# Logits by a different operand order: transposed attention rows as the stationary operand, and no folding product

## The chip, the cores and the metric

The kernel runs on one core of a Trainium2 chip. The time is the device time of the whole program in microseconds (us). In the profile the engines are PE (TensorE matmuls), PEld (TensorE weight loads), DVE (VectorE), ACT (ScalarE), POOL (GpSimd) and SP (which issues most of the DMAs).

## What is computed

Three stages follow each other. Attention with keys and values averaged over groups of 8 positions gives x (4608 tokens x 512); a soft mixture of 8 experts with 4 slots each routes tokens by `logits = x @ phi` (512 x 32); a dense layer with a softmax, a norm and an output product ends it.

```python
k_p = k.reshape(B, H, Sp, pool, D).mean(axis=3)      # B=8, H=8, S=576, D=64, Sp=72
v_p = v.reshape(B, H, Sp, pool, D).mean(axis=3)
scores = scale * np.matmul(q, k_p.transpose(0, 1, 3, 2))
attn = exp(scores - max); attn = attn / (sum + 1e-09)
x = np.matmul(attn, v_p)                             # then heads side by side: N x 512
...
logits = x @ phi                                     # N x 32
d = exp(logits - logits.max(0)); d /= d.sum(0)       # over the tokens
slot_input = d.T @ x
h = np.maximum(slot_input[e] @ w1[e], 0.0); slot_out[e] = h @ w2[e]
c = softmax(logits, over the slots); y = c @ slot_out
h = y @ w_in ... out = ln @ w_out
```

## The kernel before

x is never built. For each batch the kernel forms vphi, the product of the pooled values with phi, and takes the logits of a token as its attention row times vphi. An attention row of a token holds, for four pairs of heads, `PAIR` = 147 columns (a one, and for each head 72 probabilities and a tiny constant), 588 in all, cut into `NB` = 5 blocks of 128 (the last has 76).

A batch has 576 tokens: four tiles of 128 and one (t = 4) in which the 64 left over stand twice, half of the heads each. Tiles are numbered on through the batches. `steps` runs one step for each tile: the first batch written out, six batches in a hardware loop (two per turn), one last step, and then a tail written by hand. In the step of tile t, TensorE does, in program order, the scores of tile t + 2 (`scores`), pieces of the routing statistics of the batch before (`lmax_t`, `mb_t`, `dat_t`, `datT_t`, `slot_t`), the logits of tile t - 1 and the transposes of the attention rows of tile t (`aT_t`). Engines work in the order in which the code is written, and wait for each other by semaphores.

The part around the change, before:

- `wphi_t`: once a batch, four products phi_pair (stationary, 32 columns) by vpad (moving, 147 columns), each in its own quarter of the array's columns; ScalarE copies the four results into the wide matrix wphi (`wphi_evac`). `vphi_t` then transposes wphi in five pieces, and VectorE copies and sums them into vphi (`vphi_evac`, three instructions).
- `lt_t`: for each tile, five products with vphi (stationary, 32 columns) and the transposed attention rows aT (moving, 128 columns), spread over the four column quarters of the array, so the logits come out transposed and in four partial sums. ScalarE copies them (`lt_evac`).
- `l_t`: one product of that copy (stationary, 128 columns) with `fold4` (moving, 32 columns), which transposes back and adds the four parts. VectorE copies the result into c_all (`logit_evac`).

ScalarE's order in a step is: other copies, `lt_evac` of tile t - 1, the exponentials `exps` of tile t + 2 (they need VectorE's subtraction of the maximum, `sub_max`), and the two copies `aT_evac` of tile t. The logits of a tile need `aT_evac` of it.

Of the kernel before, what the change touches and what calls it, by code (L numbers as in the profile page):

```python
# [31 lines left out]
ALU = mybir.AluOpType  # L32
# [29 lines left out]
NB = len(BLOCKS)  # L62

# [15 lines left out]
def build(nc, q, k, v, phi, w1, w2, w_in, w_out, g_ln, out):  # L79
    with ExitStack() as ctx:  # L80
# [41 lines left out]
        wphi = bump("wphi", [P, PAIRS * PAIR])  # L122
        kblk = [bump("kblk0", [P, PAIRS, 2 * SP])]
        assert place[0] >= p1 + 2 * HALF
        lt = [bump(f"lt{i}", [P, P]) for i in range(2)]
        datT = bump("datT", [SP, 2, P])
        assert place[0] >= p1 + 2 * HALF
# [3 lines left out]
        vpad = bump("vpad", [P, PAIRS, PAIR])  # L131
# [7 lines left out]
        vphi = [bump(f"vphi{i}", [P, NB, SLOTS]) for i in range(2)]  # L139
# [12 lines left out]
        dlog = bump("dlog", [P, TILES, SLOTS])  # L152
        dexp = bump("dexp", [P, TILES + 1, SLOTS])
# [9 lines left out]
        assert (WO_EARLY - 1) * 4 * DM <= size([P, QCOLS]) and WO_EARLY == FC - 3  # L163
        for e, t in ((FC - 1, 1), (FC, 3)):
            assert wo0 + e * 4 * DM <= attn0 + 4 * (t + 1) * PAIRS * PAIR
# [5 lines left out]
        assert wo0 + size([P, FC, DM]) + HALF // 4 <= attn0 + (attn_end - attn0) // 2  # L171
        for e, t in ((4, 1), (7, 3)):
            assert wo0 + size([P, FC, DM]) + HALF * e // FC <= attn0 + (attn_end - attn0) // 2 + 4 * (t + 1) * PAIRS * PAIR
# [51 lines left out]
        b_v72, b_aT, b_lt, b_tail, b_head = ps[2], ps[3:5], ps[5], ps[6], ps[7]  # L225
# [24 lines left out]
        def weights(e, layer):  # L250

            n = 2 * e + layer
            return half(n % 10), sem(f"w_in{n % 10}"), {8: 16 * 2, 9: 16 * 4, 10: 16 * (1 + MC)}.get(n, 16 * (n // 10 + 1))
# [32 lines left out]
        def l_bank(tile):  # L286

            return ps[1] if isinstance(tile[0], int) and tile[0] == B - 1 and tile[2] == 4 else b_lt
# [42 lines left out]
        def vpad_half(hh):  # L331
            return vpad[hh * D:(hh + 1) * D, :, 1 + hh * HEAD:1 + hh * HEAD + SP]
# [51 lines left out]
        def _(sp):  # L384
# [64 lines left out]
            sp.wait_ge(sem("vphi_ps"), B)  # L449
            load_w(3, 0)  # L450
            sp.wait_ge(sem("s_ps"), B * TILES - 1)
            load_out(0, WO_EARLY - 1, 0)
            sp.wait_ge(sem("s_ps"), B * TILES)
            sp.wait_ge(sem("wphi_ps"), B)
            load_out(WO_EARLY - 1, WO_EARLY, 0)
# [3 lines left out]
            load_out(WO_EARLY, FC - 1, 1)  # L459
            sp.wait_ge(sem("dat_ps"), dat_count(B - 2, 3))  # L460
            load_out(FC - 1, FC, 1)
            sp.wait_ge(sem("dat_ps"), dat_count(B - 2, TILES - 1))
            load_part(9, 0, 2)
            sp.wait_ge(sem("lt_ps"), B * TILES)
            load_part(8, 1, 4)
            for t, a, e in ((1, 2, 4), (3, 4, 7), (4, 7, 8)):
                sp.wait_ge(sem("dat_ps"), dat_count(B - 1, t))
                load_part(9, a, e)
# [42 lines left out]
        def _(pool):  # L511
# [4 lines left out]
            pool.memset(vpad[:, :, :], 0.0).then_inc(sem("zeros"), 1)  # L516
            pool.memset(wphi[:, :], 0.0).then_inc(sem("zeros"), 1)
            pool.memset(kblk[1][:, :, :], 0.0).then_inc(sem("pool_set"), 1)
            pool.wait_ge(sem("pool_set"), 2)
            pool.wait_ge(sem("zeros"), 2)  # L520
# [118 lines left out]
        def _(act):  # L639
# [14 lines left out]
            def wphi_evac(b):  # L654

                act.wait_ge(sem("wphi_ps"), b + 1)
                for j in range(PAIRS):
                    g = 32 * GROUP[j]
                    last = copy(wphi[g:g + 32, PAIR * j:PAIR * (j + 1)], b_head[g:g + 32, 0:PAIR])
                last.then_inc(sem("wphi_sb"), 1)  # L660

# [5 lines left out]
            def lt_evac(tile):  # L667
                act.wait_ge(sem("lt_ps"), num(tile) + 1)
                o, i = lt[bit(tile)][:, :], l_bank(tile)[:, 0:P]
                if tile[2] == TILES - 1:  # L670
                    o, i = o.rearrange("p (a n) -> p a n", a=2), l_bank(tile)[:, 0:LEFT][:, None, :].to_broadcast([P, 2, LEFT])
                copy(o, i).then_inc(sem("lt_sb"), 1)
# [47 lines left out]
            act.wait_ge(sem("zeros"), 2)  # L720
# [3 lines left out]
            wphi_evac(0)  # L724
            exps((0, 0, 2))

            def step(b, par, t, first, last):
# [3 lines left out]
                if t == 5:  # L731
                    wphi_evac(b + 1)
# [12 lines left out]
                if first:  # L745
                    if t != 1:
                        lt_evac(ahead(b, par, t - 1))
# [4 lines left out]
                    if t == 1:  # L752
                        lt_evac(ahead(b, par, t - 1))
                    exps(ahead(b, par, t + 2))
                    return
                lt_evac(ahead(b, par, t - 1))
# [10 lines left out]
            lt_evac(last_tile(1))  # L767
# [3 lines left out]
            lt_evac(last_tile(2))  # L771
# [6 lines left out]
            lt_evac(last_tile(3))  # L778
            lt_evac(last_tile(4))
# [139 lines left out]
        def _(dve):  # L919
# [63 lines left out]
            def logit_evac(tile):  # L983
                dve.wait_ge(sem("l_ps"), num(tile) + 1)
                dve.tensor_copy(batch_logits(tile[0])[:, tile[2], :], l_bank(tile)[:, P:P + SLOTS]).then_inc(sem("l_sb"), 1)
# [791 lines left out]
```

## Time and profile before

| | |
|---|---|
| median of 3 runs | 441.24 us (440.08 to 441.43) |
| the profiled execution | 440.7 us, span of its instructions 438.9 us |
| busy share of the span | PE 94%, PEld 73%, DVE 70%, ACT 54%, POOL 56% |
| granted TensorE clock, mean | 0.996 of full speed |
| DMA | 91.68 MB, mean 209 GB/s |

A busy share is the union of the instructions' durations on an engine. TensorE's products overlap each other (one lasts about 0.3 us and the next starts about 0.1 us after it), so for TensorE the time from one start to the next is what an instruction takes of the engine. The span has three parts: attention and routing up to about 160 us, the experts up to about 200, and the last layer.

### The profile page before, as it was taken

What the parts mean: (1) busy time and instruction counts of PE and PEld (TensorE: products, weight loads), DVE (VectorE), ACT (ScalarE), POOL (GpSimd) and SP (SyncE); (2) the same over time, 40 slices, a digit from 0 to 9 for tenths busy, and PEclk for the clock granted to TensorE, in tenths of its full rate; (3) what the DMA queues carried; (4) which work ended last, traced back from release to release, by engine and by line L of the source; (5) the groups of instructions that cost most, each with busy time, mean ns of one, the idle gap of its engine ahead of it and who ended that gap; (6) DMA issues with size and microseconds to landing.
All of it is one profiled execution on the core that took longest, in us unless ns stands there. A gap on an engine that the chain in (4) does not pass through costs nothing.

```text
span 438.9 us, 9468 instructions
## 1 busy us (share of the span) xinstructions
PE 413.2 (94%) x3303; PEld 319.1 (73%) x3303; DVE 307.3 (70%) x543; ACT 238.8 (54%) x497; POOL 243.8 (56%) x346
## 2 busy tenths in 40 slices
PE   6788989899899889999899999999999999999997
PEld 6666777677777664455687887888888888888886
DVE  4878788787887747355889976777777777777211
ACT  1457775667756542153777655656555656555310
POOL 2579988888883311020143375757677666676540
PEclk8999999999999999999999999999999999999999
DMA  8847789769695699996001676677666666766732
GB/s 322 331 126 307 309 326 390 288 246 419 247 433 191 231 397 346 431 424 284 1 7 43 131 143 117 130 141 139 134 133 114 135 132 134 143 135 115 157 73 48
DMA packets 79212, 91.68 MB, mean 209 GB/s; under 512 B 67024, under 2 KB 67408, under 8 KB 74448
## 3 DMA queue, kind: packets, MB, share of 16 engines
q1 hardware_dynamic: 74016, 82.07, 60.9%
q10 hardware_dynamic: 5168, 9.24, 6.3%
q8 instruction: 16, 0.26, 0.2%
q14 instruction: 12, 0.10, 0.1%
HBM read 66.13 MB, written 9.44 MB: 172 GB/s over the span
## 4 chain that ended last, share of the span: by engine, by line
PE 75%; DVE 12%; ACT 5%; issue 4%; POOL 3%; DMA 1%; ACTq 0%; DVEq 0%
PE banks L1697 14%; PE banks L1698 14%; PE banks L1699 14%; PE banks L1313 5%; PE banks L1560 3%; PE banks L1669 3%; PE banks L1582 3%; PE banks L1356 2%; PE banks L1416 2%; DVE smax L960 2%; DVE attn L966 2%; DVE ssum L973 2%; PE banks L1387 2%; PE banks L1380 2%; ACT aT L641 1%
## 5 line engine op out<-in xcount | busy, mean ns | idle before, releaser
L1697 PE MATMUL banks<-wo_hi,uh 128*128 128x512 f32 x280 | 110.5, 395 | 0.1
L1698 PE MATMUL banks<-wo_lo,uh 128*128 128x512 f32 x280 | 110.0, 393 | 0.0
L1699 PE MATMUL banks<-wo_hi,ul 128*128 128x512 f32 x280 | 109.1, 390 | 0.0
L609 POOL TENSOR_TENSOR ul<-u_col,uh 128x1024 fp32r<-128x1024 f32 x30 | 71.9, 2397 | 18.6 <-ACT uh L641 18.2
L876 ACT ACTIVATE sq<-u,st 128x1024 f32<-128x1024 f32 x36 | 41.5, 1152 | 39.9 <-DVE u L1198 39.9
L533 POOL TENSOR_TENSOR attn<-attn,srec 128x576 f32<-128x576 f32 (+1 forms) x40 | 43.1, 1078 | 35.5 <-DVE srec L978 35.5
L1697 PEld LDWEIGHTS banks<-wo_hi,uh 128*128 128x128 f32 x280 | 52.6, 188 | 12.7 <-DVE ul L1215 0.5
L1699 PEld LDWEIGHTS banks<-wo_hi,ul 128*128 128x128 f32 x280 | 52.5, 188 | 12.1
L1698 PEld LDWEIGHTS banks<-wo_lo,uh 128*128 128x128 f32 x280 | 52.6, 188 | 11.3
L1198 DVE SCALAR_TENSOR_TENSOR u<-banks,ex 128x1024 f32<-128x1024 f32 x35 | 42.7, 1223 | 24.5 <-ACT ex L867 24.4
L1188 DVE TENSOR_REDUCE st<-banks 128x1 f32<-128x1024 f32 x35 | 42.6, 1216 | 18.3 <-PE banks L1669 18.3
L867 ACT ACTIVATE ex<-banks,st 128x1024 f32<-128x1024 f32 x35 | 39.0, 1115 | 18.4 <-DVE st L1188 17.7
L641 ACT ACTIVATE uh<-u_col 128x1024 fp32r<-128x1024 f32 x30 | 31.7, 1058 | 30.2 <-DMA u_col<-u_blk 16.3
L1313 PE MATMUL banks<-kblk,qb 128*128 128x144 f32 x256 | 40.6, 303 | 5.3 <-DVE attn L966 2.4
L1313 PEld LDWEIGHTS banks<-kblk,qb 128*128 128x128 f32 x256 | 34.0, 194 | 10.1 <-DVE attn L966 4.7
L1229 DVE TENSOR_SCALAR osb<-banks,rs 128x512 f32<-128x512 f32 x35 | 25.9, 741 | 19.5 <-PE banks L1699 19.5
L665 ACT ACTIVATE attn<-attn 128x576 f32<-128x576 f32 (+1 forms) x40 | 25.4, 636 | 25.5 <-DVE attn L966 25.1
L1208 DVE STREAM_TRANSPOSE u_blk<-u 128x1024 f32<-128x1024 f32 x30 | 37.4, 1246 | 1.9
L595 POOL TENSOR_SCALAR st<-st 128x1 f32<-128x1 f32 x36 | 6.9, 191 | 52.5 <-ACT sq L876 52.2
L374 POOL TENSOR_TENSOR vraw<-vraw 128x1152 f32<-128x1152 f32 (+1 forms) x14 | 29.5, 2108 | 7.4 <-DMA vraw<-in_v 7.4
L960 DVE TENSOR_REDUCE smax<-banks 128x8 f32<-128x576 f32 (+1 forms) x40 | 27.2, 680 | 8.4 <-PE banks L1313 8.4
L973 DVE TENSOR_REDUCE ssum<-attn 128x8 f32<-128x584 f32 (+1 forms) x40 | 27.8, 694 | 6.7 <-ACT attn L665 6.4
(179 smaller groups left out, 692.0 us busy)
## 6 DMA issues: line engine op xcount, KB each, us to landing
wslot<-in_moe_w SPq DMA_DIRECT2D x13, 2048.0 KB, 13.2
u_col<-u_blk SPq DMA_DIRECT2D x240, 64.0 KB, 2.2
vraw<-in_v SPq DMA_DIRECT2D x8, 1152.0 KB, 5.1
out<-osb ACTq DMA_DIRECT2D x32, 256.0 KB, 2.8
kraw<-in_k SPq DMA_DIRECT2D x7, 1152.0 KB, 7.2
qb<-in_q SPq DMA_DIRECT2D x7, 1152.0 KB, 7.6
wslot<-in_moe_w SPq DMA_DIRECT2D x4, 512.0 KB, 7.2
win<-in_moe_w_in SPq DMA_DIRECT2D x4, 512.0 KB, 22.1
```

Of the source, the lines that this page charges most:

```text
L533: pool.tensor_tensor(a, a, per_head(srec[bit(tile)], t)[:, :, :, None].to_broadcast([P, tile_pairs(t), 2, SP]), ALU.mult) \
L609: pool.tensor_tensor(ul[par][:, :, :].rearrange("p c (q t) -> p (c q) t", q=4), v, uh[par][:, :, :].bitcast(F32).rearrange("p c (q t) -> p ...
L867: act.activation(ex[par][:, :, :], h_banks(par), ACT.Exp, bias=st[k % STATS]["nmax"][:, :], accum_out=st[k % STATS]["den"][:, :]).then_inc ...
L876: act.activation(sq[par][:, :], u[k % URING][:, :], ACT.Square, scale=-float(FF), bias=st[k % STATS]["usum"][:, :], accum_out=st[k % STATS ...
L973: dve.tensor_reduce(per_head(ssum[par], t), head_sums(tile[1], t), AX.X, ALU.add).then_inc(sem("ssum"), 1)
L1188: dve.tensor_reduce(st[k % STATS]["nmax"][:, :], h_banks(k % 2), AX.XY, ALU.max, negate=True).then_inc(sem("nmax"), 1)
L1198: dve.scalar_tensor_tensor(u[k % URING][:, :].rearrange("p (a n) -> p a n", a=2), h_banks(par), 1.0, ex[par][:, :, :], ALU.mult, ALU.mult, ...
L1208: dve.transpose(u_blk[slot][:, :, :, k % 2, :].rearrange("p c q t -> p (c q) t"), u[k % URING][:, :].rearrange("p (b f) -> p b f", f=BLK)) \
L1313: last = pe.matmul(s_view[:, j, 0:2 * SP], q_cols(par, t, j), kblk[par][:, j, :], start=True, stop=True)
L1697: pe.matmul(ps[4 + par], uh[par][:, c, :], wo_hi[:, c, :], start=(c == 0), stop=False)
L1698: pe.matmul(ps[4 + par], uh[par][:, c, :], wo_lo[:, c, :], start=False, stop=False)
L1699: last = pe.matmul(ps[4 + par], ul[par][:, c, :], wo_hi[:, c, :], start=False, stop=(c == FC - 1))
```

## The change

The two operands of both products change places, and what was only there to bring the result back falls away.

- `vphi_t` takes a block of 128 columns of vpad as the stationary operand and phi_pair (32 columns) as the moving one, so vphi comes out as it is needed. For that vpad is stored with room between the pairs (`VPAD` = 147 + 128 columns a pair) so that a block of 128 can be cut at any of the five block positions; a block over two pairs takes two products that accumulate: eight in all. `wphi_t`, `wphi_evac` and the transposes are gone, and `vphi_evac` is one copy.
- The new `l_t` takes aT (128 columns) as the stationary operand and vphi (32 columns) as the moving one: five products that accumulate in one place, in the full array. For t = 4, where a tile is 64 tokens, there are twelve products in two halves of the array's columns; both halves compute the same logits, since the copies of the 64 tokens are wanted twice. The folding product, `lt_evac` and VectorE's `logit_evac` are gone; ScalarE copies the logits straight into c_all (`l_evac`).
- Some tiles move in SBUF, and a few loads of weights at the end of attention are cut in other pieces and wait for other semaphores.

```diff
-            def wphi_t(b):
+            def vphi_t(b):
                 pe.wait_ge(sem("vT_sb"), b + 1)
                 if not (isinstance(b, int) and b == 0):
                     pe.wait_ge(sem("vphi_sb"), b)
-                for j in range(PAIRS):
-                    g = 32 * GROUP[j]
-                    last = pe.matmul(b_head[g:g + 32, 0:PAIR], phi_pair[:, j, :], vpad[:, j, :], start=True, stop=True, tile_position=(0, g))
-                last.then_inc(sem("wphi_ps"), 1)
-
-            def vphi_t(b):
-
-                pe.wait_ge(sem("wphi_sb"), b + 1)
-                for n in range(1, 4):
-                    pe.transpose(b_head[:, 32 + P * (n - 1):32 + P * n], wphi[:, P * n:P * (n + 1)], ident[:, :])
...
+                for k in range(NB):
+                    pairs = [j for j in (k - 1, k) if 0 <= j < PAIRS]
+                    for j in pairs:
+                        last = pe.matmul(b_head[:, SLOTS * k:SLOTS * (k + 1)], vpad_block(j, k), phi_pair[:, j, :], start=(j == pairs[0]), stop=(j == pairs[-1]))
+                last.then_inc(sem("vphi_ps"), 1)
...
-                if t == 4:
-                    for n in range(2 * LNB):
-                        k, hh, g = n // 2, n % 2, n % 4
...
+                if t == TILES - 1:
+                    parts = [(k, hh) for hh in range(2) for k in range(LNB)]
+                    for i, (k, hh) in enumerate(parts):
                         m = BLOCKS[NB - 1] if k == LNB - 1 else P
...
+                        for c in (0, LEFT):
+                            last = pe.matmul(l_bank()[c:c + LEFT, :], aT[bit(tile)][0:m, k, LEFT * hh:LEFT * (hh + 1)], vphi[par][0:m, k + LSKIP * hh, :],
+                                             start=(i == 0), stop=(i == len(parts) - 1), tile_position=(0, c))
                 else:
                     for k, m in enumerate(BLOCKS):
-                        g = k % 4
-                        last = pe.matmul(b_lt[32 * g:32 * (g + 1), 0:P], vphi[par][0:m, k, :], aT[bit(tile)][0:m, k, :],
-                                         start=(k < 4), stop=(k + 4 >= NB), tile_position=(0, 32 * g))
-                last.then_inc(sem("lt_ps"), 1)
-
-            def l_t(tile):
-
-                pe.wait_ge(sem("lt_sb"), num(tile) + 1)
-                pe.matmul(l_bank(tile)[:, P:P + SLOTS], lt[bit(tile)][:, :], fold4[:, :], start=True, stop=True).then_inc(sem("l_ps"), 1)
+                        last = pe.matmul(l_bank(), aT[bit(tile)][0:m, k, :], vphi[par][0:m, k, :], start=(k == 0), stop=(k == NB - 1))
+                last.then_inc(sem("l_ps"), 1)
...
-            def lt_evac(tile):
-                act.wait_ge(sem("lt_ps"), num(tile) + 1)
...
+            def l_evac(tile):
+                act.wait_ge(sem("l_ps"), num(tile) + 1)
+                copy(c_all[:, bass.ds(tile[0], 1), tile[2], :].rearrange("p o s -> p (o s)"), l_bank()).then_inc(sem("l_sb"), 1)
...
             def vphi_evac(b, par):
                 dve.wait_ge(sem("vphi_ps"), b + 1)
-                dve.tensor_copy(vphi[par][:, 0, :], b_head[:, 0:32])
-                dve.tensor_reduce(vphi[par][:, 1:4, :], b_head[:, 32:32 + 3 * P].rearrange("p (k g s) -> p k s g", k=3, g=PAIRS), AX.X, ALU.add)
-                dve.tensor_copy(vphi[par][0:BLOCKS[4], 4, :], b_head[0:BLOCKS[4], 64 + 3 * P:96 + 3 * P]).then_inc(sem("vphi_sb"), 1)
+                dve.tensor_copy(vphi[par][:, :, :], b_head[:, 0:NB * SLOTS].rearrange("p (k s) -> p k s", k=NB)).then_inc(sem("vphi_sb"), 1)
```

TensorE's program in the loop, from the transposes of tile t = 4 to those at the end of a batch. Names are outputs and inputs, the numbers behind them are buffers, and the shape is that of the output. Before:

```order
L1352 MATMUL banks<-ident,attn 128x64 x6
L1387 MATMUL banks<-fold_50,lt_69 128x32
L1425 MATMUL banks<-ident,dat 72x128 x2
L1323 MATMUL banks<-vpad,phi_pair 32x147 x4
L1297 REGISTER_ALU
L1313 MATMUL banks<-kblk_75,qb_72 128x144 x4
L1434 MATMUL banks<-v_1_83,datT 32x64 x8
L1364 ISA
L1375 MATMUL banks<-aT_78,vphi_80 32x64 x6
L1356 MATMUL banks<-ident,attn 128x128 x4
```

The kernel before goes on from there, to the end of the batch:

```order
L1356 MATMUL banks<-ident,attn 76x128
L1387 MATMUL banks<-fold_50,lt_68 128x32
L1340 MATMUL banks<-ident,vT_77 72x128 x4
L1330 MATMUL banks<-ident,wphi 128x128 x3
L1331 MATMUL banks<-ident,wphi 128x32
L1332 MATMUL banks<-ident,wphi 76x64
```

The same place of the changed program:

```order
L1386 MATMUL banks<-ident,dat 72x128 x2
L1274 REGISTER_ALU
L1290 MATMUL banks<-kblk_66,qb_62 128x144 x4
L1395 MATMUL banks<-v_0_81,datT 32x64 x8
L1333 ISA
L1343 MATMUL banks<-vphi_80,aT_79 64x32 x12
L1326 MATMUL banks<-ident,attn 128x128 x4
L1326 MATMUL banks<-ident,attn 76x128
L1310 MATMUL banks<-ident,vT_76 72x128 x4
L1301 MATMUL banks<-phi_pair,vpad 128x32 x8
```

The folding products (L1387), the four products of L1323 and the five transposes of wphi are gone; twelve products of 64 x 32 stand where six of 32 x 64 stood, and eight of 128 x 32 stand at the end of the batch.

ScalarE's program in the step of t = 5 of a batch (the first tile of the next one), from the copy datT to the copies of aT. Before:

```order
L641 ACTIVATE datT<-banks 72x256
L641 ACTIVATE wphi<-banks 32x147 x4
L641 ACTIVATE lt_69<-banks 128x128
L664 REGISTER_ALU
L665 ACTIVATE attn<-attn 128x4x2x72
L675 ISA
L641 ACTIVATE aT_78<-banks 128x512
L675 REGISTER_ALU
L641 ACTIVATE aT_78<-banks 76x128
```

The changed one:

```order
L643 ACTIVATE datT<-banks 72x256
L643 ISA
L643 ACTIVATE c_all<-banks 128x32
L658 REGISTER_ALU
L659 ACTIVATE attn<-attn 128x4x2x72
L666 ISA
L643 ACTIVATE aT_78<-banks 128x512
L666 REGISTER_ALU
L643 ACTIVATE aT_78<-banks 76x128
```

The wphi copies are gone, and the copy of the logits stands where the copy lt stood, ahead of the exponentials (`attn<-attn`).

## Rows read from the trace of the kernel before

**Rows 1.** Table by stretch, attention loop: window, its length, each engine's busy us, clock, DMA

```profile
38.00:145.50 107.50, 99.91 (x1280) 78.44 (x1280) 86.64 (x205) 72.76 (x210) 85.33 (x65) 1.00 0.76 303
```

**Rows 2.** Timeline of TensorE, first steps of a batch: start us, length us, what [idle before]

```profile
75.18 0.60 PE L1380 MATMUL banks<-aT,vphi 128*32 128x128 f32 x10
75.71 0.77 PE L1356 MATMUL banks<-ident,attn 128*128 128x128 f32 x5
76.31 0.31 PE L1387 MATMUL banks<-fold,lt 128*128 128x32 f32 x2
77.11 0.71 PE L1309 MATMUL banks<-kblk,qb 128*64 128x144 f32 x8 [0.49 <-DVE attn L966]
78.47 0.63 PE L1380 MATMUL banks<-aT,vphi 128*32 128x128 f32 x10 [0.65 <-ACT aT L641]
...
80.50 1.24 PE L1313 MATMUL banks<-kblk,qb 128*128 128x144 f32 x8 [0.22 <-issue]
```

**Rows 3.** Timeline of TensorE, the rest of the same batch

```profile
82.19 0.60 PE L1380 MATMUL banks<-aT,vphi 128*32 128x128 f32 x10
82.73 0.77 PE L1356 MATMUL banks<-ident,attn 128*128 128x128 f32 x5
...
83.78 0.96 PE L1416 MATMUL banks<-attn,dexp 128*32 128x147 f32 x24
84.67 1.25 PE L1313 MATMUL banks<-kblk,qb 128*128 128x144 f32 x8
85.85 0.63 PE L1380 MATMUL banks<-aT,vphi 128*32 128x128 f32 x10
86.41 0.41 PE L1352 MATMUL banks<-ident,attn 64*128 64x64 f32 x6
86.84 0.41 PE L1387 MATMUL banks<-fold,lt 128*128 128x32 f32 x2
87.09 0.39 PE L1425 MATMUL banks<-ident,dat 128*72 128x128 f32 x2
...
87.79 1.25 PE L1313 MATMUL banks<-kblk,qb 128*128 128x144 f32 x8
...
89.25 0.42 PE L1375 MATMUL banks<-aT,vphi 128*32 128x64 f32 x12
89.60 0.76 PE L1356 MATMUL banks<-ident,attn 128*128 128x128 f32 x5
...
90.57 0.61 PE L1340 MATMUL banks<-ident,vT 128*72 128x128 f32 x4
91.01 0.49 PE L1330 MATMUL banks<-ident,wphi 128*128 128x128 f32 x3
91.43 0.24 PE L1331 MATMUL banks<-ident,wphi 32*128 32x32 f32 x1
...
91.79 0.39 PE L1313 MATMUL banks<-kblk,qb 128*128 128x144 f32 x1
```

**Rows 4.** Timeline of TensorE, four products of the last stage's preparation

```profile
205.45 1.08 PE L1628 MATMUL banks<-fold,so 128*128 128x32 f32 x8 [0.20 <-DVE so L1172]
```

**Rows 5.** The same line by itself: duration ns min/median/max, first and last start

```profile
L1628 PE MATMUL banks<-fold,so x8: 276/276/297, 205.4 to 206.3; 128*128 128x32 f32 x8
```

**Rows 6.** Timeline of ScalarE, the exponentials of the batch's second step

```profile
75.82 0.28 ACT L641 ACTIVATE lt<-banks 128x128 f32<-128x128 f32 x1 [0.98 <-PE banks L1380]
77.09 0.68 ACT L665 ACTIVATE attn<-attn 128x576 f32<-128x576 f32 x1 [1.00 <-DVE attn L966]
```

**Rows 7.** Timeline of VectorE, the copies into vphi

```profile
73.86 0.19 DVE L989 COPY vphi<-banks 128x32 f32<-128x32 f32 x1 [0.29 <-PE banks L1332]
...
74.53 0.75 DVE L973 TENSOR_REDUCE ssum<-attn 128x8 f32<-128x584 f32 x1
```

**Rows 8.** Timeline of TensorE, end of the first batch and of the attention stage

```profile
36.34 0.73 PE L1356 MATMUL banks<-ident,attn 128*128 128x128 f32 x5 [0.55 <-POOL attn L533]
...
158.43 0.43 PE L1396 MATMUL banks<-ident,lmax 128*32 128x128 f32 x8 [0.40 <-DVE lmax L997]
```

More of the change, by code:

```diff
@@ L62 @@
 NB = len(BLOCKS)
+VPAD = PAIR + P
 LPAIRS = PAIRS // 2
@@ L121, in build @@
         kp = bump("kp", [P, PAIRS, SP])
-        wphi = bump("wphi", [P, PAIRS * PAIR])
         kblk = [bump("kblk0", [P, PAIRS, 2 * SP])]
-        assert place[0] >= p1 + 2 * HALF
-        lt = [bump(f"lt{i}", [P, P]) for i in range(2)]
+        vphi = [bump("vphi0", [P, NB, SLOTS])]
+        place[0] = p1 + 2 * HALF
         datT = bump("datT", [SP, 2, P])
+        dlog = bump("dlog", [P, TILES, SLOTS])
+        dexp = bump("dexp", [P, TILES + 1, SLOTS])
         assert place[0] >= p1 + 2 * HALF
@@ L138, in build @@
         aT = [bump(f"aT{i}", [P, NB, P]) for i in range(2)]
-        vphi = [bump(f"vphi{i}", [P, NB, SLOTS]) for i in range(2)]
+        vphi.append(bump("vphi1", [P, NB, SLOTS]))
         assert place[0] <= attn_end + HALF
@@ L162, in build @@
         WO_EARLY = (attn0 - wo0) // (4 * DM)
-        assert (WO_EARLY - 1) * 4 * DM <= size([P, QCOLS]) and WO_EARLY == FC - 3
-        for e, t in ((FC - 1, 1), (FC, 3)):
-            assert wo0 + e * 4 * DM <= attn0 + 4 * (t + 1) * PAIRS * PAIR
+        assert WO_EARLY == FC - 2 and wo0 + FC * 4 * DM <= attn0 + 4 * 2 * PAIRS * PAIR
         wten = bump("wten", [P, 4 * FF])
@@ L168, in build @@
         place[0] = attn_end
[L171 to L173 removed]
+        ten = attn0 + (attn_end - attn0) // 2 - (wo0 + size([P, FC, DM]))
+        assert 4 * 4 * DM <= ten
+        for e, t in ((6, 1), (8, 3)):
+            assert e * 4 * DM <= ten + 4 * (t + 1) * PAIRS * PAIR
         wnine = at("wnine", [P, 4 * FF], F32, attn_end)
@@ L284, in last_tile, with l_bank @@
             return B - 1, 1, t
-        def l_bank(tile):
-            return ps[1] if isinstance(tile[0], int) and tile[0] == B - 1 and tile[2] == 4 else b_lt
+        def l_bank():
+            return b_l[:, 0:SLOTS]
         def tile_pairs(t):
@@ L746, in step @@
                     if t != 1:
-                        lt_evac(ahead(b, par, t - 1))
+                        l_evac(ahead(b, par, t - 1))
                     if t == 4:
@@ L1060, in step @@
                         slot_acc(b - 1, 1 - par)
-                logit_evac(ahead(b, par, t - 1))
                 if t == 5:
@@ L1461, in step @@
                     dat_t(b - 1, 1 - par, (4,))
-                if t == 1 and first:
-                    wphi_t(b)
-                if t == 5 and first:
-                    wphi_t(b + 1)
                 if not (last and t + 2 >= TILES):
@@ L1476, in step @@
                     vphi_t(b)
+                    pe.wait_ge(sem("aT_sb"), 2)
                     aT_t(tile)
-                lt_t(before, first and t == 1)
+                l_t(before, first and t == 1)
                 if t == 2 and not first:
@@ L1486, in step @@
                     dat_t(b - 1, 1 - par, (0, 1))
-                l_t(before)
                 if t == 2 and first:
@@ L1494, in step @@
                         datT_t(b - 1)
-                if t == 4 and not last and not first:
-                    wphi_t(b + 1)
                 if t == 5:
```

98 lines of the change are left out of this document (32 added, 66 removed).

## The prediction

> **What bounds the kernel now.** I read the table by stretch first: in the attention loop TensorE is busy 99.9 of 107.5 us at full clock, VectorE 86.6, the others less [rows 1]. All that the change touches lies in this stage. Busy time of TensorE can hide waits, though, so I read its timeline next, from start to start. In the shown batch (one turn of the loop holds two) it waits visibly in three places only: 0.49 us for VectorE's subtraction, 0.65 for ScalarE's copy aT, 0.22 at the next scores [rows 2]. From 80.50 to 91.79 it goes from one piece of work to the next with no idle shown [rows 2, 3]. So what a change adds to TensorE's work there comes out in full, and what it takes from VectorE or ScalarE is worth only what it shortens of those waits.
>
> **The unit prices.** In the trace each product of the program (not a transpose) has two rows, so the five products of a tile are ten rows. The new product, 128 columns of f32 stationary and 32 moving, stands in the trace in just this form: four of them in a row last 1.08 us as eight rows, one row lasting 0.28 [rows 4, 5], so the rows follow each other every (1.08 - 0.28)/7 = 0.114 us. Five products take 1.14 us, the eight of vphi 16 x 0.114 = 1.82. The old group of five takes 0.54 from its start to the next work (82.19 to 82.73), since four column quarters work at once; at 85.85 it takes 0.56 [rows 3]. Both hold the step back from narrow columns to the full array. I price such a change of shape from two neighbours: four transposes take 90.57 to 91.01, 0.11 each; three more, followed by one of another row shape, take 0.42, so the change costs 0.42 - 0.33 = 0.09 [rows 3].
>
> The twelve products of t = 4 are not in the trace in their form. They are 24 rows in 12 pairs, the two column halves together. Upper bound for a pair: the scores in the same two halves, four pairs with 144 moving columns, 0.71 us with about 0.28 for the last, so (0.71 - 0.28)/3 = 0.14 a pair [rows 2]. Lower bound: half of the 0.114, if the time goes with the stationary columns, 64 instead of 128. With 32 moving columns the form is nearer to that one; I take 0.057, hence 0.68 for twelve.
>
> The Trainium skill ("TensorE: Matmul & The Clock Gate", Back-to-back issue gap) gives some 81 ns for a sustained stream of weight loads and 128-column products, where the row above has 114. By the page's figure the change would come out otherwise; I price that as a rival and keep the row for the sum.
>
> **The change step by step, for one batch of the loop.** I go through TensorE's places in order of time.
>
> 1. First two tiles, up to 80.50. The logits group at 75.18 follows narrow work: it costs the change of shape earlier, 0.09, and 1.14 instead of 75.18 to 75.71: +0.69. The folding product is gone: -0.25 (its place 86.84 to 87.09) [rows 2, 3]. That is +0.44, and the wait of 0.49 behind it takes it up if VectorE is earlier. It is: its three copies into vphi take 73.86 to 74.53, 0.67 [rows 7]; one copy costs at least the 0.19 of a fifth of its columns and at most those 0.67, so I take 0.25 and VectorE comes 0.4 sooner. The scores stay at about 77.1. The next group waits for ScalarE, where the exponentials (77.09, released by VectorE) stand ahead of the copy aT [rows 6]. There a new wait appears: the copy of the logits stands ahead of the exponentials, and the logits of this tile now end at 75.18 + 0.09 + 1.03 + 0.28 = 76.58; with a copy of 0.2 (bounds 0.19, the vphi copy of the same shape, and 0.28, the old one) the exponentials can start at 76.85, not 0.4 but 0.24 sooner. So the group at 78.47 starts at 78.23, takes 0.6 to 0.7 longer, and the 0.22 wait and one folding product (0.25) are given back: 80.4 to 80.5. No change; since the loop's other batch waits less there, I take +0.05.
> 2. Up to 84.67. The group at 82.19 follows narrow work: +0.69. From the transposes at 82.73 to 83.78 there are 1.05 us, for five transposes (0.60, as 75.71 to 76.31) and a change of shape (0.09) once the folding product and its wait for ScalarE's copy go [rows 2, 3]: -0.36. Sum +0.33.
> 3. Up to 87.79. The scores no longer end in a change of shape, -0.09. The group at 85.85 takes 1.14 for 0.56, and 0.09 to change to the half-row transposes: +0.67. Folding product -0.25. From datT (87.09) to the next scores 0.70 us go down to two transposes, 0.24, without the wphi products and their two changes of shape: -0.46 [rows 3]. Sum -0.13.
> 4. Up to 91.79. The t = 4 group, 0.35 from 89.25 to 89.60, becomes 0.68 + 0.18 for two changes of shape, +0.51. Transposes and folding product, 89.60 to 90.57, 0.97 to 0.60: -0.37. The transposes of wphi, 91.01 to 91.79, 0.78, against 1.82: +1.04 [rows 3]. Sum +1.18.
>
> The batch becomes 0.05 + 0.33 - 0.13 + 1.18 = 1.4 us longer. VectorE loses five small copies a batch and ScalarE four wphi copies; both are hidden behind TensorE already and bring nothing more.
>
> **Where it counts.** Six batches run in the loop: 8.5. In the first batch TensorE waits for POOL and VectorE in most steps, as at 36.34 (0.55 of idle) [rows 8], and that takes up the longer groups; behind that wait there are the vphi products, +1.04, less the place of one folding product, of which I take 0.14, a row or so, since nothing waits for it there: +0.9. In the tail after 145.5 four more groups follow. The first starts 0.24 sooner and is 0.7 longer, the next two add some 0.6 each and lose a folding product (0.25 each); the last (t = 4) adds 0.4 and must wait for ScalarE's copies of transposes that now come just before it. That is 0.5 + 0.3 + 0.3 + 0.4 plus about 0.6 of wait, against one wait that shrinks: before, 158.43 came after two folding products and two copies behind the last group [rows 8], and one product and one copy, 0.3 or so, go. I take +1.8. The expert stage and the last layer do the same work as before; the weight loads cut anew are tied to work that itself comes later, and attention gives them more time.
>
> Sum: 8.5 + 0.9 + 1.8 = 11.2 us on the profiled execution's own 440.7 (span 438.9), so 451.9. The median of the runs is 0.5 above that execution: **452.4 us**.
>
> **The rivals.**
>
> - *Forecast*: added TensorE time comes out as summed, 449.7 to 455. Chance 0.60.
> - *Waits give more back.* The 0.65 wait at 78.47 [rows 2] goes too, if the logits copy doesn't hold up the exponentials. For it: VectorE is 0.4 sooner. Against: the order on ScalarE. 7 x 0.65 = 4.6 less, about 447.8. With small errors of the unit price, 0.17.
> - *The half-column pairs go at 0.14*, not 0.057: 12 x 0.083 = 1.0 a batch, or ScalarE's late copies push out every step. Up to 8 us more, 455 to 460. Against: only 32 columns move. Chance 0.15.
> - *Faster than before*: weight loads of 128 columns run ahead under the work before, so the new rows follow more closely than 0.114. The trace has a hint: two rows of the folding product right behind transposes last 0.31 together, elsewhere 0.41 (76.31 and 86.84) [rows 2, 3], so the second came 0.10 earlier. It decides where 56 rows of this form a batch (four tiles of ten and sixteen for vphi) save the 1.4 us: at 1.4/56 = 0.025 less, 0.089 a row. At 0.08 a batch would be 0.034 x 56 - 1.4 = 0.5 shorter, some 3.5 us over seven batches with the tail even: 438. Against it: rows 4 and 5, a run of eight with every load free to run ahead, hold 0.114. Chance 0.05.
> - *No change*: all waits, 0.49 + 0.65 + 0.22 = 1.36 a batch, take up the 1.4. Steps 2 to 4 have no wait to do that. Chance 0.03.
>
> The page's 81 ns for such a stream would be the fourth of these, nearly at its 0.08. The same skill ("TensorEngine Tiling (Array Packing)", When to Use Tiling) advises what the kernel did before: with 32 moving columns, swap the operands and use four column tiles. By the rows that is right here, since five products take 0.54 so and 1.14 the other way.
>
> **How the numbers follow.** A range of 447.5 to 457 holds the forecast case, most of the second and the lower part of the third, a little over 8 in 10. What a measurement can tell from no change here is about 0.3%, 1.3 us. Faster 0.05, same 0.03, slower 0.92.
>
> **What would show it.** In the changed profile the logits rows (128 x 32) should start every 0.11, five products taking 1.1 us; the vphi products 1.8 us at the end of a batch; t = 4 about 0.7. A turn of the loop, two batches, should be 2.8 us longer. TensorE's wait for VectorE at the scores of t = 4 should be gone, the wait for ScalarE behind it should remain at about 0.6. Experts and last layer should keep their lengths. I am wrong if the rows of the new form come closer than 0.09, if the pairs take over 0.1, or if the steps from 80.50 on hold a wait that busy time hid from me.

## The result and the profile after

| | before | changed |
|---|---|---|
| median | 440.66 us (439.25 to 441.43, 4 runs) | 460.13 us (453.50 to 465.28, 4 runs) |
| ratio | | 1.0341, 95% interval 1.0248 to 1.0434 |
| profiled execution | 440.7 us, span 438.9 | 462.7 us, span 460.9 |
| mean granted clock of TensorE | 0.996 (profiled) | 0.966 (profiled); 0.989, 0.959, 0.978 in the others |

The ratio leaves out the two runs with the lowest clocks. The program is slower, as forecast. The two runs that the ratio keeps have a mean of 455.5 us, 3.1 above the forecast of 452.4 and inside the range; the median of all four lies 7.7 us above the forecast and above the top of the range, and the four times of one program lie 12 us apart. They are ordered by the clock: 453.50 us at 0.989, 457.55 at 0.978, 462.72 at 0.966, 465.28 at 0.959, some 3.9 us for each 0.01. So there are two things to read: what the change costs where the clock is full, and where the clock falls.

**Where the clock falls.** The row of the granted clock on the page of the changed kernel, over 40 slices of 11.5 us:

```profile
PEclk9985599999999998999999999999999999999999
```

and the same row of the kernel before:

```profile
PEclk8999999999999999999999999999999999999999
```

The table by stretch of the changed kernel (window, its length, busy us of PE, PEld, DVE, ACT, POOL, then the clock):

```profile
25.00:30.00 5.00, 3.65 (x30) 3.31 (x29) 3.57 (x6) 3.00 (x8) 2.52 (x2) 1.00 0.41 170
30.00:35.00 5.00, 5.00 (x29) 4.82 (x28) 2.84 (x6) 1.88 (x7) 4.38 (x4) 0.53 0.82 302
35.00:55.00 20.00, 20.00 (x115) 17.94 (x115) 8.49 (x19) 6.58 (x18) 11.23 (x10) 0.50 0.60 233
55.00:60.00 5.00, 5.00 (x60) 3.81 (x59) 1.78 (x3) 2.68 (x8) 2.30 (x1) 0.74 0.89 375
126.00:164.50 38.50, 37.38 (x439) 32.72 (x438) 26.88 (x54) 20.89 (x61) 22.39 (x19) 1.00 0.57 229
164.50:185.00 20.50, 18.00 (x229) 12.82 (x232) 8.69 (x21) 6.83 (x25) 3.61 (x6) 0.92 0.90 329
```

From about 30 to 57 us TensorE runs at the lower of its two levels, 1.2 instead of 2.4 GHz, and while it is there it is busy all the time: 5.00 of 5, 20.00 of 20. Reading busy shares alone one would see an engine at its limit; the counts give it away, 115 rows in 20 us against 439 in 38.5. TensorE's timeline there:

```profile
26.36 1.20 PE L1347 MATMUL banks<-vphi,aT 128*128 128x32 f32 x10
27.67 0.74 PE L1326 MATMUL banks<-ident,attn 128*128 128x128 f32 x5
29.65 1.71 PE L1290 MATMUL banks<-kblk,qb 128*128 128x144 f32 x8 [1.25 <-DVE attn L954]
31.16 2.18 PE L1347 MATMUL banks<-vphi,aT 128*128 128x32 f32 x10
33.27 0.59 PE L1322 MATMUL banks<-ident,attn 64*128 64x64 f32 x6
...
39.41 3.46 PE L1301 MATMUL banks<-phi_pair,vpad 128*128 128x32 f32 x16
42.68 2.27 PE L1290 MATMUL banks<-kblk,qb 128*128 128x144 f32 x8
```

What came before the fall: five logits products of the new form, five transposes, 1.25 us of waiting for VectorE's subtraction, and the first of eight rows of scores, which last 1.71 us together where the same eight take 1.25 at full clock. The next logits group takes 2.11 us to its successor (31.16 to 33.27), the vphi products 3.27.

**At full clock** the timeline of TensorE over a whole batch, the fifth of the loop's six:

```profile
126.00 1.23 PE L1290 MATMUL banks<-kblk,qb 128*128 128x144 f32 x8
127.16 0.42 PE L1357 MATMUL banks<-ident,lmax 128*32 128x128 f32 x8
127.51 1.30 PE L1347 MATMUL banks<-vphi,aT 128*128 128x32 f32 x10
128.65 0.74 PE L1326 MATMUL banks<-ident,attn 128*128 128x128 f32 x5
129.32 0.71 PE L1286 MATMUL banks<-kblk,qb 128*64 128x144 f32 x8
130.43 1.30 PE L1347 MATMUL banks<-vphi,aT 128*128 128x32 f32 x10 [0.39 <-ACT aT L643]
...
132.59 1.15 PE L1290 MATMUL banks<-kblk,qb 128*128 128x144 f32 x8
...
137.01 1.25 PE L1290 MATMUL banks<-kblk,qb 128*128 128x144 f32 x8
...
139.89 1.25 PE L1290 MATMUL banks<-kblk,qb 128*128 128x144 f32 x8
141.31 0.43 PE L1395 MATMUL banks<-v,datT 72*32 72x64 f32 x16 [0.17 <-ACT datT L643]
141.67 0.89 PE L1343 MATMUL banks<-vphi,aT 128*64 128x32 f32 x24
142.49 0.77 PE L1326 MATMUL banks<-ident,attn 128*128 128x128 f32 x5
...
143.53 1.87 PE L1301 MATMUL banks<-phi_pair,vpad 128*128 128x32 f32 x16
145.24 0.37 PE L1290 MATMUL banks<-kblk,qb 128*128 128x144 f32 x1
...
164.47 1.23 PE L1290 MATMUL banks<-kblk,qb 128*128 128x144 f32 x8
```

Starts are read here, and not lengths: a logits group goes from 127.51 to 128.65, 1.14 us; at t = 4 the group takes 0.82 (141.67 to 142.49); vphi takes 1.71 (143.53 to 145.24). The wait for VectorE at the scores of t = 4 [rows 2] is gone (129.32 has none), the one for ScalarE is 0.39, and there is a small new one, 0.17, for ScalarE's copy datT. In the kernel before, the batch of [rows 2] and [rows 3], also the first of its turn, began 1.42 us ahead of the first row of [rows 2], at 73.76:

```profile
73.76 1.25 PE L1313 MATMUL banks<-kblk,qb 128*128 128x144 f32 x8
```

It ended at 91.79 [rows 3]. So this batch takes 19.24 us for 18.03. The two batches of a turn take 38.47 (126.00 to 164.47) for 35.87 (73.76 to 109.63): +2.60 a turn, +1.3 a batch.

### The profile page after: what moved, and what is told of

The parts are those of the page before. It is cut to its first block, busy times and chain, and to the rows that moved or that the text cites. A ratio compares the mean times of both kernels' runs of the same rounds, so it can differ in the third digit from the quotient of the medians.

```text
span 460.9 us, 9460 instructions
## 1 busy us (share of the span) xinstructions
PE 442.5 (96%) x3343; PEld 355.8 (77%) x3343; DVE 299.4 (65%) x487; ACT 226.9 (49%) x465; POOL 243.9 (53%) x345
## 4 chain that ended last, share of the span: by engine, by line
PE 81%; DVE 8%; ACT 5%; issue 3%; POOL 2%; DMA 1%; ACTq 0%; DVEq 0%
PE banks L1648 13%; PE banks L1647 13%; PE banks L1649 13%; PE banks L1347 7%; PE banks L1290 6%; PE banks L1326 3%; PE banks L1510 3%; PE banks L1301 3%; PE banks L1619 3%; PE banks L1532 3%; PE banks L1377 3%; ACT aT L643 2%; DVE attn L954 2%; DVE smax L948 2%; PE banks L1343 2%
## 5 line engine op out<-in xcount | busy, mean ns | idle before, releaser
L1347 PEld LDWEIGHTS banks<-vphi,aT 128*128 128x128 f32 (+1 forms) x320 | 41.5, 205 | 8.8 <-ACT aT L643 6.0
L1290 PE MATMUL banks<-kblk,qb 128*128 128x144 f32 x256 | 42.6, 313 | 4.9 <-DVE attn L954 3.4
L1347 PE MATMUL banks<-vphi,aT 128*128 128x32 f32 (+1 forms) x320 | 44.0, 287 | 3.0 <-ACT aT L643 3.0
L1290 PEld LDWEIGHTS banks<-kblk,qb 128*128 128x128 f32 x256 | 36.2, 205 | 8.8 <-DVE attn L954 5.5
L643 ACT ACTIVATE c_all<-banks 128x32 f32 (+1 forms) x40 | 7.9, 197 | 68.4 <-PE banks L1347 56.8
```

What stands on the lines that cost most here:

```text
L643: return act.activation(o, i, ACT.Copy, scale=scale)
L1290: last = pe.matmul(s_view[:, j, 0:2 * SP], q_cols(par, t, j), kblk[par][:, j, :], start=True, stop=True)
L1347: last = pe.matmul(l_bank(), aT[bit(tile)][0:m, k, :], vphi[par][0:m, k, :], start=(k == 0), stop=(k == NB - 1))
```

## Experiments

Both theories below take it that the rows of the new form cost the summed 10 or 11 us and that the rest is the clock. **A**: the clock falls because TensorE sits idle at its waits. **B**: it falls because products that move only 32 columns for each load of 128 leave the array nearly empty, however busy the engine looks. Ratios are to the kernel before on the same chip, which had medians of 441.4, 441.8 and 440.2 us.

### Work in the gaps at the start

The kernel has a helper for such gaps, `keep_clock(bank, n)`, n transposes of the identity whose result nobody reads. Ten instead of three stand at t = 1 of the first batch, and twelve are new at t = 4.

```diff
                 if t == 1 and first:
-                    keep_clock(b_tail, 3)
+                    keep_clock(b_tail, 10)
+                if t == 4 and first:
+                    keep_clock(b_tail, 12)
```

> The changed kernel with 19 more transposes of the identity in the first batch, at two places where TensorE waits (about 1.0 us before the scores of tile 3 and 1.25 us before those of tile 6). Theory A (the clock falls after the first batch because TensorE sits idle there): no stretch at half clock behind 25 us, every run at 450 to 452.5, runs within 1 us of each other. Theory B (it falls because the new products keep the array nearly empty while its weight loads run): the fall comes later or in some runs only, times still scatter from 452 to 463. If the clock has nothing to do with the 8 us above the forecast, the time stays near 460.

Measured: 453.45 us (451.03 to 457.41), ratio 1.028 (1.020 to 1.0359). The clock is full from 25 to 60 us (33.54 busy of 35). Two runs at 0.996 take 451.11 and 451.03, two at 0.985 and 0.978 take 455.78 and 457.41. In the profiled one the clock now falls behind the loop. The row of its page, and below it TensorE's timeline there:

```profile
PEclk9999999999999966999999999999999999999999
```

```profile
158.31 1.30 PE L1347 MATMUL banks<-vphi,aT 128*128 128x32 f32 x10 [0.28 <-ACT aT L643]
...
161.38 2.34 PE L1347 MATMUL banks<-vphi,aT 128*128 128x32 f32 x10 [0.74 <-ACT aT L643]
163.53 1.31 PE L1326 MATMUL banks<-ident,attn 128*128 128x128 f32 x5
```

So there is a second weak place, the tail, where the same groups stand between waits. That work in the gap at the start helps is likely and not shown: two of four runs have a mean clock of 0.996, which none of the eight runs of the unedited changed kernel reaches, but the repeat below keeps its clock at the start without it. "Every run at 450 to 452.5", A's outcome, did not come true; the fall that comes later, or in some runs only, is B's. A repeat of the unedited changed kernel:

> The changed kernel once more, for the scatter. Both theories: runs between 450.5 and 466, and the later ones are those with the lower mean clock: about 4.3 us more for each 0.01 of clock lost.

Measured: 460.0 us (456.32 at clock 0.981 to 468.33 at 0.949), ratio 1.0422 (1.0344 to 1.0499). That is 3.8 us for each 0.01 of clock and not 4.3, and one run lies above the 466 expected. In this profile the clock stays up at the start and is 0.50 from 170 to 175 us, in the tail. Which weak place gives way changes from one execution to the next.

### The same products, moving four times the columns

The logits product of a full tile moves vphi four times over, 128 columns, into 128 columns of the same bank; nothing reads the last 96. Loads, waits and order stay.

```diff
-                        last = pe.matmul(l_bank(), aT[bit(tile)][0:m, k, :], vphi[par][0:m, k, :], start=(k == 0), stop=(k == NB - 1))
+                        last = pe.matmul(b_l[:, 0:4 * SLOTS].rearrange("p (r s) -> p r s", r=4), aT[bit(tile)][0:m, k, :],
+                                         vphi[par][0:m, k, :][:, None, :].to_broadcast([m, 4, SLOTS]), start=(k == 0), stop=(k == NB - 1))
```

> The changed kernel, in which the logits products of the four full tiles move vphi four times over (128 columns instead of 32) into spare columns of the bank; the output is the same. Rows of the form stay bound by their weight load, so 0.11 us each and 0 us on a batch at full clock. Theory B (a nearly empty array lets the clock fall): the clock stays up, 450 to 452.5 in every run. Theory A (idle time does it): nothing changes, half clock from about 30 to 57 us in some form, 453 to 465.

Measured: 453.53 us (452.71 to 454.10), ratio 1.0289 (1.0256 to 1.0322), clocks 0.992 to 0.996. More work, and the clock is at 0.992 or more in all four runs, where the changed kernel has 0.949 to 0.989 in eight. The median is 6.6 us below the changed kernel's; beside the two runs that the changed kernel's ratio keeps (455.5) it is 2.0 below. The rest is the runs at low clock, which the wide form does not have. TensorE's timeline at the place where the changed kernel's clock fell:

```profile
26.59 1.28 PE L1347 MATMUL banks<-vphi,aT 128*128 128x128 f32 x10
27.83 0.74 PE L1326 MATMUL banks<-ident,attn 128*128 128x128 f32 x5
29.82 1.25 PE L1290 MATMUL banks<-kblk,qb 128*128 128x144 f32 x8 [1.25 <-DVE attn L954]
30.90 1.28 PE L1347 MATMUL banks<-vphi,aT 128*128 128x128 f32 x10
```

The wait is the same 1.25 us, and the clock holds: 1.00 from 0 to 60 us. Waiting alone is not what lets it fall. The median is above the expected 450 to 452.5, since a wide group takes a little longer than a narrow one (a turn of the loop 38.9 us for 38.5) and a short dip in the tail stays, 0.67 from 170 to 175 us.

### Each half alone

Only `vphi_t` in its new form (eight products with vpad stationary, one copy), the logits, folding product and `lt_evac` as before:

> Only the vphi half of the change; the logits by four column quarters, copy and folding product as before. By the places of the forecast a batch of the loop takes +0.46 to +0.58 us against the kernel before (1.7 to 1.8 of products for 0.78 of transposes and 0.46 of wphi): 3.5 us over the whole, 444 to 445.5. A rival who holds that VectorE's shorter copy is what counts expects 439 to 440.

Measured: 444.61 us (443.26 to 446.26), ratio 1.0098 (1.0059 to 1.0137), clocks 0.988 to 0.999; a turn of the loop takes 36.62 us, +0.4 a batch. The expected 444 to 445.5 holds, and the rival's 439 to 440 does not.

Only the logits in their new form, wphi, its copies and its transposes as before:

> Only the logits half of the change; vphi by wphi and transposes as before. A batch of the loop takes +0.85 us: about 7 us with the tail, 447 to 449 at full clock; more, and scattered, if the clock falls at the start as in the full change. If the two halves add up, e3 and e4 together give the full change at full clock, +10 to +11.

Measured: 455.44 us (449.32 at 0.992 to 462.71 at 0.959); no ratio, since its runs lie too far apart. A turn takes 37.40, +0.77 a batch. The halves add up to 1.14 of the full change's 1.3, and the scatter comes with the logits half. In its profiled execution the clock dips to 0.70 from 45 to 50 us, and again in the tail. So the loop's first batch is a third weak place.

### The cost at full clock

The fills at the start, 13 more transposes at three places of the tail, and the wide form in the first batch and the tail only; the loop is that of the changed kernel.

```diff
             aT_t(last_tile(2))
+            pe.wait_ge(sem("v72_sb"), B)
+            keep_clock(ps[2], 5)
             l_t(last_tile(2))
...
+            keep_clock(ps[2], 3)
             l_t(last_tile(4))
+            keep_clock(ps[2], 5)
             datT_t(B - 2, ps[0])
```

> The changed kernel with fillers at the waits of the first batch (19 transposes of the identity) and of the tail (13), and with the logits products of the first and the last batch moving 128 columns (32 of them wanted); the loop is the changed kernel's own. Theory B (emptiness of the array together with waits lets the clock fall at both ends of the attention stage): all runs within 1.5 us at 450.5 to 452, clock 0.99 or more. If the fall could come in the loop as well, a run in four or so lies above 453.

Measured: 450.36 us (449.98 to 450.77), ratio 1.0207 (1.0178 to 1.0235), clocks 0.996 to 1.000. The scatter is gone, and this is about what the change costs when the clock does not fall; the fillers and the wide groups, which stand in its time too, cannot add much, since the two runs of the first experiment at 0.996 take 451.03 and 451.11. The table by stretch over the tail, filler included:

```profile
160.00:185.00 25.00, 24.16 (x347) 14.99 (x349) 12.37 (x29) 8.69 (x27) 2.69 (x6) 1.00 0.96 353
```

### The copy of the logits behind the exponentials

The rival "waits give more back" says that the copy into c_all holds the exponentials up. Here ScalarE takes them first, in the kernel of the last section.

```diff
-                l_evac(ahead(b, par, t - 1))
                 if not (last and t + 2 >= TILES):
                     exps(ahead(b, par, t + 2))
+                l_evac(ahead(b, par, t - 1))
```

> e6 with the exponentials ahead of the logits copy on ScalarE. The rival of the forecast (the wait for ScalarE at the second group goes if the copy doesn't stand in front): 4 us less than e6. My reading of the changed profile, where the exponentials start 0.08 us after VectorE is done: 0 to 0.5 us less.

Measured: 451.54 us (450.30 to 452.05), ratio 1.0221 (1.0189 to 1.0253), 1.2 above the unswapped one, for an expected 0 to 0.5 below. Most of the 1.2 is the clock. In the profiled execution, 452.05 us at 0.996, it falls for a short while in the loop's first batch, in spite of the fillers at both ends:

```profile
42.55 1.30 PE L1348 MATMUL banks<-vphi,aT 128*128 128x32 f32 x10 [0.45 <-ACT aT L643]
...
44.83 2.12 PE L1290 MATMUL banks<-kblk,qb 128*128 128x144 f32 x8
```

The eight rows of scores last 2.12 for 1.25. The swapped run at 0.999 takes 450.30, between the unswapped ones at 0.999, 450.17 and 450.56. So the swap gains nothing, and the loop of narrow products is not quite safe either.

TensorE's wait for ScalarE at the second group, in a batch that begins at 116.94, is 0.43 in place of 0.39. Why is seen on ScalarE's timeline there:

```profile
119.94 0.69 ACT L659 ACTIVATE attn<-attn 128x576 f32<-128x576 f32 x1 [3.04 <-DVE attn L954]
```

The row shows that even first in line the exponentials start 3.00 us into the batch; in the changed kernel it is 3.05, so the copy ahead of them costs 0.05. VectorE's subtraction sets the time, as its own timeline in the changed kernel says (batch from 126.00):

```profile
126.20 0.32 DVE L973 COPY vphi<-banks 128x160 f32<-128x160 f32 x1 [1.80 <-PE banks L1301]
126.44 0.75 DVE L961 TENSOR_REDUCE ssum<-attn 128x8 f32<-128x584 f32 x1
...
128.21 0.76 DVE L954 TENSOR_TENSOR attn<-banks,smax 128x576 f32<-128x576 f32 x1
```

The subtraction ends at 128.97, and ScalarE's copy and exponentials go at once:

```profile
128.95 0.20 ACT L643 ACTIVATE c_all<-banks 128x32 f32 x1 [2.98 <-PE banks L1347]
129.05 0.68 ACT L659 ACTIVATE attn<-attn 128x576 f32<-128x576 f32 x1
```

### Twice the logits products, narrow and wide

A stronger test of B in the loop, where TensorE waits little. In the kernel with the clock held up the loop moves 32 columns a product, and its clock stays up:

```profile
100.00:150.00 50.00, 48.66 (x574) 42.52 (x575) 34.52 (x71) 28.07 (x83) 33.27 (x27) 1.00 0.72 286
```

Now each full tile makes its five products twice, once into another part of the bank.

```diff
+                    for k, m in enumerate(BLOCKS):
+                        pe.matmul(b_l[:, 256:256 + SLOTS], aT[bit(tile)][0:m, k, :], vphi[par][0:m, k, :], start=(k == 0), stop=(k == NB - 1))
```

> e6 with the five logits products of each full tile made twice, the first time into unused columns of the bank (32 tiles, 320 more rows of 128 x 32). At 0.114 us a row, with about 2 to 4 us taken up by waits in the first batch and at the second tile of each batch: +32 to +35 us on e6. If weight loads could run ahead and a row took 0.08: +22 to +25.

Measured: 497.43 us (484.00 at clock 0.995 to 506.12 at 0.949). The run at 0.995 is 33.6 above the kernel without the second set, close to the sum at 0.114 a row. Then the same, with both sets moving 128 columns everywhere:

> e8 with both sets of logits products of the full tiles moving 128 columns instead of 32. A row then takes 0.123 us instead of 0.114, so the time at full clock is some 5 us above e8's fastest run, 487 to 490. Theory B (the emptiness of the array lets the clock fall): the clock stays at 0.99 or more and all runs lie within 2 us, so the median is under e8's 497 although each row takes longer. If it is the number of weight loads in a row that does it, or the waits, the clock falls as in e8 and the runs scatter from 487 to 510.

Measured: 484.94 us (484.67 to 485.12), ratio 1.1014 (1.0977 to 1.1052), clock 0.996 in all four. Four times the columns moved, and 12.5 us less in the median. All of the 12.5 is in the three narrow runs at 0.949 to 0.969: the narrow one at 0.995, 484.00, is 0.9 below the wide median. The table by stretch of the narrow kernel:

```profile
100.00:150.00 50.00, 49.20 (x475) 43.77 (x473) 23.39 (x48) 20.65 (x61) 26.33 (x21) 0.83 0.57 225
```

and of the wide one:

```profile
100.00:150.00 50.00, 49.14 (x546) 44.37 (x539) 28.23 (x56) 22.10 (x66) 31.97 (x23) 1.00 0.63 250
```

TensorE is busy 49.20 of 50 us in one and 49.14 in the other, the weight loads 43.8 and 44.4; only the columns moved differ, and the clock is 0.83 or 1.00. The narrow kernel's timeline catches a fall; L1347 is the first set of a tile and L1350 the second:

```profile
101.44 1.30 PE L1347 MATMUL banks<-vphi,aT 128*128 128x32 f32 x10 [0.39 <-ACT aT L643]
102.58 1.56 PE L1350 MATMUL banks<-vphi,aT 128*128 128x32 f32 x10
...
108.95 2.34 PE L1347 MATMUL banks<-vphi,aT 128*128 128x32 f32 x10
111.10 1.25 PE L1350 MATMUL banks<-vphi,aT 128*128 128x32 f32 x5
```

One set takes 1.14 us before (101.44 to 102.58) and the last one 2.15 (108.95 to 111.10). The fall comes in the second set of the first tile, and here too a wait stands shortly before it, of 0.39. In the wide kernel the first set takes 1.21 and the second 1.12:

```profile
100.18 1.38 PE L1347 MATMUL banks<-vphi,aT 128*128 128x128 f32 x10
101.39 1.28 PE L1351 MATMUL banks<-vphi,aT 128*128 128x128 f32 x10
102.51 0.71 PE L1326 MATMUL banks<-ident,attn 128*128 128x128 f32 x5
```

The expected 487 to 490 was too high, since the second wide set costs no more than a narrow one; that the scatter would be under 2 us came true. Waits alone, theory A, fall with the two pairs: order and semaphores are the same in both doubled programs, and so are they in the changed kernel and its wide form. The doubled pair ran on two different chips, the changed kernel's repeat and its wide form on one.

The runs taken together say the same. Of the 20 runs with narrow logits products and either no fillers at one of the two ends or the products doubled (the changed kernel, its repeat, the first experiment, the logits half, the doubled narrow one), 15 have a mean clock below 0.988. Of the 41 others that the experiments list (21 of the kernel before on both chips, 4 of the vphi half, 8 of the wide ones, 8 with the clock held up), none has.

## Why the prediction was right, and where it failed

Where the time went, by places in the profiled executions (us; each difference against before; "clock held up" is the kernel with fillers and wide products at both ends of the stage):

| part | before | forecast | clock held up | changed |
|---|---|---|---|---|
| start to the loop | 38.27 | +0.9 | -0.3 | +4.4 |
| six batches of the loop | 107.23 | +8.5 | +8.2 | +14.6 |
| from there to the first expert product | 20.48 | +1.8 | +2.2 | +3.5 |
| the rest | 272.9 | 0 | -0.7 | -0.5 |
| span | 438.9 | +11.2 | +9.3 | +22.0 |

**The sign and the full-clock sum were right.** With the clock held up the profiled execution is 9.3 us above before, for 11.2 forecast, and the median of 450.36 is 2.0 below the forecast's 452.4. That the runs kept by the ratio, 455.5, lie inside the range is in part luck: its upper part was made for half-column pairs at 0.14, and it was the clock, which no term prices, that brought them there.

- *Unit prices.* A group of five products takes 1.14 us, as forecast from [rows 4, 5]. The first group of the batch starts 1.51 after the batch (126.00 to 127.51), before 1.42: the 0.09 for the change of shape. t = 4 takes 0.82 in place of 0.35, and the v products in front of it 0.36 (141.31 to 141.67) for 0.27, the change of shape: +0.56 for the forecast +0.51. That is 12 pairs at 0.068 at most, so the half columns go near the lower bound of 0.057 and not at 0.14. VectorE's one copy takes 0.24 to the next instruction (126.20 to 126.44), for 0.25. Mis-sized: vphi at 1.71, not 1.82, as sixteen rows of 0.107 each.
- *Steps of the batch*, measured against forecast: up to the second scores -0.15 (+0.05), then +0.25 (+0.33), -0.24 (-0.13), +1.35 (+1.18). The last holds the new 0.17 wait for datT, which the prediction did not have: the change removes the wphi products that had stood between datT's copy and its use, and the vphi half alone shows the same 0.17. The sum is 1.21 for this batch and 1.39 for the loop's other one (145.24 to 164.47, before 91.79 to 109.63), 1.3 for the forecast 1.4, or 2.60 a turn for 2.8.
- *The waits.* VectorE's 0.49 went as forecast. The exponentials start 3.05 after the batch, before 77.09 - 73.76 = 3.33: 0.28 sooner, forecast 0.24. The group behind them starts 4.43 after the batch, before 4.71, again 0.28 sooner, while the scores ahead of it end where they did (4.03 after the batch, before 4.06). So the recorded wait shrank from 0.65 to 0.39. The sign "about 0.6" did not follow from the prediction's own working, in which the group moves to 78.23 behind scores that stay, a wait of 0.41. The reason given for 0.24 and not 0.4, the copy of the logits ahead of the exponentials, was right for 0.05 of it only: the swap starts them 0.05 sooner. The subtraction itself ends 0.33 sooner and not 0.4 (2.97 after the batch, before 3.30), because VectorE's copy of vphi starts 0.10 later in the batch, behind longer vphi products.
- *First batch.* -0.3 for +0.9 with the clock held up. This term can't be judged closely: the kernel before has a stretch of low clock of its own at the start, in its table by stretch

```profile
5.00:10.00 5.00, 2.70 (x17) 2.49 (x16) 3.00 (x7) 0.44 (x1) 0.00 (x0) 0.86 1.02 424
10.00:15.00 5.00, 4.66 (x32) 4.41 (x31) 3.22 (x6) 0.69 (x1) 3.33 (x2) 0.80 1.03 414
```

  which the profiled executions of the changed one and of the one with the clock held up do not have, worth at most 5 x 0.14 + 5 x 0.20 = 1.7 us. The 9.3 of the whole is too small by as much at most.
- *Tail.* +2.2 for +1.8, but with 13 filler transposes in it.
- *Experts and last layer* kept their lengths, as forecast, within 0.7 us.

**The step that failed** is the missing term for the clock: "added TensorE time comes out as summed", on top of a loop read "at full clock" [rows 1]. It took the full clock as given for the new work, and "what would make it wrong" named row spacing, pairs and hidden waits, not the clock. In the changed kernel about 12.7 us (22.0 less 9.3) of the profiled execution came from there: 4.7 in the first batch, 6.4 in the loop (all in its first batch, up to where the clock comes back), 1.3 in the tail. The form was in the row already used for the price [rows 4], 32 columns moved for each 128 loaded, where the old group moved 128 in four quarters at once. That row stands at full clock, and I had read it for its spacing only; nothing in the trace before shows what five such products in every step do.

The rule of the Trainium skill ("TensorE: Matmul & The Clock Gate", HAM oscillation) tells of pauses between matmuls as what lets the engine be throttled. The traces here agree only in part: the falls come behind waits, of 1.25 us in the changed kernel, 0.45 in the swapped one and 0.39 in the doubled one, but the same 1.25 us wait in the wide kernel lets nothing fall, and the doubled kernel's clock is 0.83 where it is busy 49.20 of 50.

**The rivals.** "Waits give more back" (447.8) is refuted by the swap. The half-column pairs at 0.14 are refuted by the 0.82; the 455.5 of the kept runs lies in that rival's 455 to 460, but not by its cause. "Faster", by rows closer than 0.089, is refuted by the 1.14 us of ten rows in every trace at full clock. "No change" is refuted by the loop. The 81 ns of the Trainium skill ("TensorE: Matmul & The Clock Gate", Back-to-back issue gap) don't hold here: the page gives them for 128 moving columns, and the traces have 0.107 to 0.114 us for rows with 32 and 0.112 to 0.121 for rows with 128.

**What stays open.** The runs tell narrow from wide products, and not whether it is the columns moved, the share of the array's work that they make, or something else that goes with them. Nor do they tell why narrow products in a loop with a wait of 0.39 a batch hold the clock at 1.00 in one profiled execution and let it dip in another, or why one execution falls at the start and the next in the tail. None of the kernels tried beats the one before: the whole change with the clock held up is 2.1% slower, the vphi half alone 1.0%.

## What to carry to other kernels

A product that loads 128 columns and moves 32 took about as long here as one that loads and moves 128 (1.14 us for five, and 1.12 to 1.21): five took that 1.14 us where the same five with the operands swapped, 32 columns stationary in four quarters and 128 moving, took 0.54. A folding product of 0.25 and two copies are a good price for that: the logits half alone costs 0.77 us a batch. Before added TensorE time is priced at full clock, ask how many columns the new products move for each load; where they moved few, in every step and between waits, the clock fell here and single runs scattered, so read each time beside its clock. A cheap test is to move more columns than are needed: if the runs come together at a higher clock, the scatter was the clock's.

## What was not expected of the hardware

- TensorE's granted clock fell to 1.2 GHz after waits of 0.39 to 1.25 us, and stayed there while it was busy 20.00 of 20 us (0.50 over 35 to 55 us of the changed kernel); over 100 to 150 us of the doubled one it was 0.83 at 49.20 busy of 50. Moving 128 columns in place of 32 with the same loads held it at 1.00 in both stretches, and the doubled kernel's runs then lie at 484.67 to 485.12 us in place of 484.00 to 506.12.
- Four times the moving columns cost a group 0.08 us or nothing at full clock: ten narrow rows 1.14 (101.44 to 102.58), ten wide ones 1.21 (100.18 to 101.39), and the ten wide ones behind those 1.12 (101.39 to 102.51). What sets the pace of such a row is hardly the columns moved.
- At 1.2 GHz the spacing of these rows nearly doubles too, 2.11 us for ten in place of 1.14.
- The same program varies by 12 us (453.50 to 465.28) over 0.030 of mean clock; the kernel before stays within 2.4 us in each of its sets of runs.
